# The second mixture of experts of an attention and two-MoE kernel: routing, folding of the weights, and staging

## The reference, cut to what matters

```
c = exp(logits - logits.max(1)); c /= c.sum(1)        # 3072 x 32
x = c @ slot_out                                      # soft MoE, 3072 x 512
logits = x @ w_gate                                   # 512 x 8
expert_idx = argmax(logits, axis=1)
gate_w = softmax(logits)[arange(N), expert_idx]
for e in range(8):
    mask = expert_idx == e
    if not mask.any(): continue
    out[mask] = gate_w[mask, None] * (np.maximum(x[mask] @ w1[e], 0) @ w2[e])
```

## Time and profile before

| | |
|---|---|
| median of 3 runs | 523.89 us (521.55 to 524.42) |
| the profiled execution | 521.48 us |
| its span, first to last instruction | 519.4 us |
| TensorE busy | 472.0 us (91%) |
| VectorE, ScalarE, GpSimd busy | 236.9, 222.9, 203.8 us |
| mean granted TensorE clock | 0.951 of full |
| read from HBM, written | 94.11 MB, 8.13 MB |

### The profile page before, as it was taken

The page is one execution under the profiler, slowest core; times in us unless marked ns, Lnnn a source line. Parts: engine busy times, 40 slices in busy tenths (PEclk is TensorE's granted clock), DMA queues, the critical chain, the costliest instruction groups (busy, mean ns, idle before and its releaser), DMA issues. The chain is left out here.

```text
span 519.4 us, 9980 instructions
## 1 busy us (share of the span) xinstructions
PE 472.0 (91%) x3247; PEld 378.9 (73%) x3248; DVE 236.9 (46%) x783; ACT 222.9 (43%) x442; POOL 203.8 (39%) x183
## 2 busy tenths in 40 slices
PE   8799999999999799899958997579999999999962
PEld 8599999999999777455524242458888888888842
DVE  5467777777777534631112950413333333333352
ACT  1578778778777443210101766412222222222231
POOL 2888888898985001010000001013333333333312
PEclk9999999999999989989995999679999999999977
DMA  6599899867651096599999960443333333333321
GB/s 235 207 414 387 317 370 333 334 236 261 232 190 59 8 368 278 212 392 401 408 415 409 410 229 5 130 169 128 130 132 131 131 132 131 131 132 131 130 66 49
DMA packets 38069, 116.37 MB, mean 224 GB/s; under 512 B 4304, under 2 KB 4304, under 8 KB 38032
## 3 DMA queue, kind: packets, MB, share of 16 engines
q1 hardware_dynamic: 27104, 92.28, 46.9%
q10 hardware_dynamic: 7632, 13.90, 6.9%
q0 software_dynamic: 3296, 9.70, 5.4%
HBM read 94.11 MB, written 8.13 MB: 197 GB/s over the span
## 5 line engine op out<-in xcount | busy, mean ns | idle before, releaser
L431 ACT ACTIVATE Pb<-Pb,nm 128x256 f32<-128x256 f32 (+1 forms) x192 | 83.7, 484 | 33.3 <-DVE nm L532 33.3
L378 PE MATMUL O<-V,PTs 128*128 128x65 f32 x704 | 90.2, 269 | 1.1 <-ACT PTs L457 1.1
L1335 PE MATMUL Gp<-w2h,hh 128*128 128x512 f32 x200 | 85.8, 429 | 5.8 <-DVE w2l L1570 4.9
L378 PEld LDWEIGHTS O<-V,PTs 128*128 128x128 f32 x704 | 86.4, 191 | 2.4 <-ACT PTs L457 1.3
L532 DVE CUSTOM_DVE_ANT_0 Pb<-S,TA 128x256 f32<-128x256 f32 (+1 forms) x192 | 68.7, 396 | 36.4 <-PE S L351 34.4
L1336 PE MATMUL Gp<-w2l,hh 128*128 128x512 f32 x200 | 80.3, 401 | 0.0
L1337 PE MATMUL Gp<-w2h,hl 128*128 128x512 f32 x200 | 80.2, 401 | 0.0
L1386 ACT ACTIVATE hh<-Gp 128x512 fp32r<-128x512 f32 x51 | 30.6, 600 | 109.2 <-PE Gp L1290 104.3
L1214 POOL DMA_INDIRECT Cg<-c_rows,src x28 | 27.5, 984 | 102.3 <-PE Cp L1284 100.5
L309 POOL TENSOR_TENSOR kl<-k_raw,kh 128x1632 fp32r<-128x1632 f32 x15 | 55.2, 3681 | 8.5 <-ACT kh L441 8.3
L360 PE MATMUL PT<-ident,Pb 128*128 128x128 f32 x352 | 55.2, 275 | 2.1 <-ACT Pb L431 2.1
(11 more groups left out here) (229 smaller groups left out, 655.2 us busy)
## 6 DMA issues: line engine op xcount, KB each, us to landing
mem<-in_moe_w SPq DMA_DIRECT2D x20, 2048.0 KB, 14.1
Gst<-Gall ACTq DMA_DIRECT2D x53, 256.0 KB
k_raw<-in_k SPq DMA_DIRECT2D x16, 816.0 KB, 8.2
q_raw<-in_q SPq DMA_DIRECT2D x16, 768.0 KB, 6.7
ext<-in_moe_w SPq DMA_DIRECT2D x6, 2048.0 KB, 17.9
V<-in_v SPq DMA_DIRECT2D x16, 715.0 KB, 5.4
c_rows<-XL POOLq DMA_DIRECT2D x1, 1536.0 KB, 13.8
Cg<-c_rows,src POOLq DMA_INDIRECT x28
```

Of the source, the lines that this page charges most:

```text
L378: mm = pe.matmul(O[grp % 2][:, at:at + VC], PTs[:, par, (h * kbs + kb) * P:(h * kbs + kb + 1) * P], V[:, buf, h, vb, :], start=(n == 0), s ...
L431: nc.scalar.activation(Pb[:, par, h, 0:width(g)], Pb[:, par, h, 0:width(g)], ACT.Exp, bias=nm[:, par, h:h + 1], scale=-1.0).then_inc(exp_d ...
L1335: pe.matmul(Y, hh[:, fc, :], w2h[:, cols], start=(fc == 0), stop=False)
```

## The change

Folding is moved behind the routing and done only for the experts that have tokens, from the list of them. SP loads no v1 in the soft block; when the list is known it loads the v1 of each active expert into one of two slots, then the first w2. Folding uses full matmuls that add the four chunks up in PSUM, with the replicated `STR`, so joining and its copy fall away, and the low rows are made by VectorE from PSUM. G is kept by the rank of the expert, and comes to the stage by ScalarE copies instead of DMAs. Counts come from column sums before the matmul (8 columns instead of 192), running sums from scans. The sort is two passes, first the token index, later the two gate columns; `OB` is made in 24 operations, and `OB` and `OW` have buffers of their own. The first three gathers take their index without a copy. `busy(n)` are n matmuls of 128 columns whose result nobody reads. A tiny load of w_gate only serves the semaphore count.

```diff
-        for e in range(XSLOTS - 1 + MEMW):
-            sp.wait_ge(piece_used, MEMW + EXT + e + 1)
-            load_v1(sp, e)
...
+        busy(3)
         pe.wait_ge(y_out, 1)
...
         mm.then_inc(st_done, 1)
+        busy(3)
...
-    Gall = sb(st, "Gall", [P, NE, F], F32R)
+    Gall = mem[:, 2:4, :].rearrange("p a (b f) -> p (a b) f", f=F)
-    OB = w2l[:, 0:TT * P].rearrange("p (t c) -> p t c", c=P)
-    OW = w2h[:, 0:TT * 3 * MAXT].rearrange("p (t a b) -> p t a b", a=3, b=MAXT)
+    OB = sb(st, "OB", [P, TT, P], F32R)
+    OW = sb(st, "OW", [P, TT, 3, MAXT], F32R)
...
+    def v1_slot(r):
+        return mem[:, MEMW + r, :] if isinstance(r, int) else mem[:, bass.ds(MEMW + r, 1), :].rearrange(
+            "p a f -> p (a f)")
+    def load_v1(sp, e, r, done):
+        sp.dma_start(v1_slot(r).rearrange("p (c f) -> p c f", c=DC),
+                     v1_d[bass.ds(e, 1)].rearrange("a (c p) f -> p (a c) f", p=P)).then_inc(done, 16)
     @block.sync
     def _(sp):
-        for e in range(2):
-            sp.wait_ge(gp_done, 2 * e + 2)
-            load_v1(sp, NE - 2 + e)
-        sp.wait_ge(gp_done, 6)
-        sp.wait_ge(rt_ready, 1)
-        load_v2(sp, entry(sp, 0, 0))
+        sp.dma_start(spare[:, 0:DC * NE].rearrange("p (c s) -> p c s", c=DC),
+                     wg_d.rearrange("(c p) s -> p c s", p=P)).then_inc(v1_rest, 16)
+        sp.wait_ge(experts_known, 1)
+        load_v1(sp, entry(sp, 0, 0), 0, v1_first)
         used = count(sp)
         with sp.If(used > 1):
             with sp.Fori(1, used) as r:
                 e = entry(sp, r, 0)
+                sp.wait_ge(v1_rest, r * 16)
+                sp.sem_inc(sp_passed, 1)
+                sp.wait_ge(gp_done, r * 2)
+                sp.sem_inc(sp_passed, 1)
+                load_v1(sp, e, r % 2, v1_rest)
+        load_v2(sp, entry(sp, 0, 0))
+        with sp.If(used > 1):
+            with sp.Fori(1, used) as r:
+                e = entry(sp, r, 0)
                 sp.wait_ge(w2_low, r * W2CH)
                 sp.sem_inc(sp_passed, 1)
                 load_v2(sp, e)
...
+        pool.sem_inc(gp_done, 2)
+        pool.sem_inc(g_low, 2)
         pool.wait_ge(src_ready, 1)
         def gather(u, turned):
...
-            nc.gpsimd.tensor_copy(src1[:], src_i[:, bass.ds(column(u), 1)]).then_inc(src_copied, 1)
-            pool.wait_ge(src_copied, u + 1)
+            if isinstance(u, int):
+                index = src_i[:, u:u + 1]
+            else:
+                index = src1[:, 0:1]
+                nc.gpsimd.tensor_copy(src1[:], src_i[:, bass.ds(column(u), 1)]).then_inc(src_copied, 1)
+                pool.wait_ge(src_copied, u - 2)
...
             nc.gpsimd.indirect_dma_start(out=Cg[:], out_offset=None, in_=c_dram,
-                                         in_offset=bass.IndirectOffsetOnAxis(ap=src1[:, 0:1], axis=0)
+                                         in_offset=bass.IndirectOffsetOnAxis(ap=index, axis=0)
                                          ).then_inc(gathered, 16)
         for u in range(3):
             gather(u, u)
+        pool.wait_ge(rt_ready, 1)
+        pool.wait_ge(dst_ready, 1)
...
+        def busy(count):
+            for _ in range(count):
+                pe.matmul(Cp[:, 0:P], ident[:], ones[:], start=True, stop=True)
+        def sort(which, cols):
+            for t in range(TT):
+                if t % REP == 0:
+                    pe.wait_ge(hot_done, t // REP + 1)
+                mm = pe.matmul(Sp[:, cols], OB[:, t, :], OW[:, t, which].rearrange("p a b -> p (a b)"),
+                               start=(t == 0), stop=(t == TT - 1))
+            mm.then_inc(sorted_done, 1)
...
         mm.then_inc(gw_done, 1)
+        busy(3)
         pe.wait_ge(gw_out, 1)
...
         mm.then_inc(l2_done, 1)
-        pe.wait_ge(nident_done, 1)
-        units(range(0, 2))
+        busy(9)
         pe.wait_ge(oh_done, 1)
         pe.wait_ge(lt_done, 1)
-        pe.matmul(Rp, lt[:], oh[:].rearrange("p t e -> p (t e)"), start=True, stop=True)
-        pe.matmul(Tp, ones[:], oh[:].rearrange("p t e -> p (t e)"),
-                  start=True, stop=True).then_inc(ranks_done, 1)
-        units(range(2, 2 * (NE - 2)))
-        for t in range(TT):
-            if t % REP == 0:
-                pe.wait_ge(hot_done, t // REP + 1)
-            mm = pe.matmul(Sp[:, 0:3 * MAXT], OB[:, t, :], OW[:, t].rearrange("p a b -> p (a b)"),
-                           start=(t == 0), stop=(t == TT - 1))
-        mm.then_inc(sorted_done, 1)
-        units(range(2 * (NE - 2), UNITS + 2))
+        pe.matmul(Rp, lt[:], cnt[:], start=True, stop=True)
+        pe.matmul(Tp, ones[:], cnt[:], start=True, stop=True).then_inc(ranks_done, 1)
+        busy(28)
+        sort(slice(0, 1), slice(0, MAXT))
+        pe.wait_ge(v1_first, 16)
+        used = count(pe)
+        with pe.Fori(0, used) as r:
+            pe.wait_ge(v1_rest, (r + 1) * 16)
+            pe.wait_ge(g_low, r * 2 + 2)
+            slot = v1_slot(r % 2)
+            for half in range(2):
+                for c in range(DC):
+                    at = c * F + half * 512
+                    mm = pe.matmul(Gp[:, half, :], STR[:, c].rearrange("p r s -> p (r s)"), slot[:, at:at + 512],
+                                   start=(c == 0), stop=(c == DC - 1))
+                mm.then_inc(gp_done, 1)
         turn(0)
         pe.wait_ge(cgt_out, 1)
+        pe.wait_ge(g_low, used * 2 + 2)
         for half in range(2):
             hidden(0, half)
-        with pe.Fori(0, count(pe)) as rank:
+        pe.wait_ge(gates_hot, 1)
+        sort(slice(1, 3), slice(MAXT, 3 * MAXT))
+        pe.wait_ge(rt_ready, 1)
+        with pe.Fori(0, used) as rank:
...
+        act.wait_ge(r_shifted, 1)
+        nc.scalar.activation(E2[:], T2[:], ACT.Exp).then_inc(r_exp, 1)
+        act.wait_ge(experts_known, 1)
+        used = count(act)
+        with act.Fori(0, used) as r:
+            for half in range(2):
+                act.wait_ge(gp_done, r * 2 + half + 3)
+                nc.scalar.copy(Gall[:, bass.ds(r, 1), half * 512:(half + 1) * 512].rearrange(
+                    "p a f -> p (a f)").bitcast(F32R), Gp[:, half, :]).then_inc(g_high, 1)
...
         def fetch(e, half):
             cols = slice(half * 512, (half + 1) * 512)
-            act.dma_start(Gst[:, cols].bitcast(F32),
-                          Gall[:, bass.ds(e, 1), cols].rearrange("p a f -> p (a f)").bitcast(F32)).then_inc(g_here[half], 16)
+            g = Gall[:, e, cols] if isinstance(e, int) else Gall[:, bass.ds(e, 1), cols].rearrange("p a f -> p (a f)")
+            nc.scalar.copy(Gst[:, cols], g).then_inc(g_here[half], 1)
         act.wait_ge(rt_ready, 1)
-        act.wait_ge(g_low, 2 * NE)
-        e0 = act.value_load(te[0:1, 0:1], min_val=0, max_val=NE - 1)
-        for half in range(2):
-            fetch(e0, half)
-        act.wait_ge(v2_loaded, 16)
-        act.wait_ge(sorted_done, 1)
-        for ch in range(W2CH):
+        e1 = act.value_load(tr[0:1, 1:2], min_val=0, max_val=NE - 1)
+        act.wait_ge(g_low, used * 2 + 2)
+        act.sem_inc(act_passed, 1)
+        def second_high(ch):
+            act.wait_ge(v2_loaded, 16)
             nc.scalar.copy(w2h[:, chunk(ch)], raw[:, chunk(ch)]).then_inc(w2_high, 1)
+        fetch(0, 0)
         turned_out(0)
-        e1 = act.value_load(te[0:1, 1:2], min_val=0, max_val=NE - 1)
+        fetch(0, 1)
+        second_high(0)
         relu(0, 0)
         fetch(e1, 0)
-        used = count(act)
+        for ch in range(1, W2CH):
+            second_high(ch)
...
-        total = all_tiles(act)
-        for half in range(2):
-            act.wait_ge(g_here[half], (total + 2 - half) * 16)
-        act.sem_inc(act_passed, 1)
...
+        dve.wait_ge(gw_done, 1)
+        v.tensor_tensor(GWs[:], GWp.unsqueeze(1).to_broadcast([P, REP, NE]),
+                        own_rows[:].unsqueeze(2).to_broadcast([P, REP, NE]), ALU.mult).then_inc(gw_out, 1)
...
         dve.wait_ge(l2_done, 1)
+        L2 = L2p.rearrange("p (t e) -> p t e", e=NE)
+        step(v.tensor_reduce(m2[:], L2, AX, ALU.max))
+        v.tensor_tensor(T2[:], L2, over_experts(m2[:]), ALU.subtract).then_inc(r_shifted, 1)
         dve.wait_ge(r_shifted, 1)
+        step(v.scalar_tensor_tensor(T1[:], T2[:], 0.0, over_tiles(ex[:]), ALU.is_equal, ALU.mult))
         step(v.tensor_reduce(m2[:], T1[:], AX, ALU.min))
+        step(v.tensor_tensor(by_tile(oh[:]), over_experts(m2[:]), over_tiles(ex[:]), ALU.is_equal))
+        v.tensor_reduce(cnt[:], oh[:], AX, ALU.add).then_inc(oh_done, 1)
+        v.tensor_tensor_scan(flat(cum[:]), flat(keep[:]), flat(oh[:]), 0.0, ALU.mult, ALU.add)
         dve.wait_ge(ranks_done, 1)
+        v.tensor_scalar(nt_i[:, 0, :], Tp, float(P - 1), None, ALU.add)
+        step(v.tensor_scalar(act[:], Tp, 0.0, None, ALU.is_gt))
+        v.tensor_scalar(nt_i[:, 1, :], nt_i[:, 0, :], 7, None, ALU.logical_shift_right)
+        step(v.tensor_tensor_scan(order[:], keep[:, 0, 1:1 + NE], act[:], 0.0, ALU.mult, ALU.add))
...
```

(38 more changed lines are left out.)

222 lines of the change are left out of this document (53 added, 169 removed).

## The result

The median is 505.08 us (four runs, 501.17 to 507.07) against 524.15 us (four runs, 521.55 to 528.09) before, a ratio of 0.962 with an interval of 0.953 to 0.971. Run again in five rounds, the changed kernel has 502.97 us against 523.92, a ratio of 0.959 (0.953 to 0.965); one of these six runs, 506.50, counts as slow and is left out of the ratio. So the change makes the kernel faster, by 19 to 21 us between medians; 26 us in the span and 27 between medians had been forecast.

What follows compares the result with a forecast made beforehand. Bounds named: the soft-MoE barrier, folding all eight experts and the loop's entry, then TensorE's 6.49 us tile pitch. Loop start 309.3 + 1.7 first tile + 2.7 clock = 313.7, against 339.9, saves 26.2: span 493.2, forecast 496.5 us, range 491 to 505.

Steps and rivals of the forecast that it cites:

- Block end: End of the soft MoE: without the six v1 loads the barrier follows VectorE at 268.8 us, saving 5.5.
- router: From the block's end to the list of experts: steps sum to 7.8 us, experts known at 276.6, not 293.4.
- Load: First expert's v1 after the list: 7.6 us from issue to landing, landed at 285.05.
- Sorting beside it: VectorE's positions, one-hot products and OB during the load: OB 3.6 us, index pass ends at 285.1, level with the load.
- rival (b): Chain of list, load and fold longer than priced, by slow landing or OB pieces of 0.21: 500 to 503 us; chance 0.15.
- This change escapes: Cutting OB into 24 pieces avoids the skill's fixed-cost warning: 0.13 us a piece by its table, 3.0 in all.
- Fold: Two listed experts on TensorE: 6.9 us each with 1.5 after each, both G's whole at 302.75.
- Entry of the loop: From folded weights to the tile loop: ScalarE 4.6 us, VectorE 1.2 and 0.7; loop starts at 309.3.
- First tile: First tile of the loop: w2 chunks and register loads delay it, ending near 317.5 instead of 315.8; loss 1.7 us.
- Clock: Granted clock falling ahead of the fold and ahead of the loop: an allowance of 2.7 us.
- Rival (a): Clock lost for most of the fold: 509 to 511 us at half clock throughout, 503 with half of it; chance 0.10.
- Stage copies: ScalarE's two copies of 0.58 us replacing two DMA issues of 0.5 in the steady loop, costed at nothing.

Runs made afterwards that it cites:

- Experiment 1: Kernel before the change, with only the fifth and sixth v1 loads moved from the soft block to the head of the last block: 518.39 us against 525.69.
- experiment 7: Changed kernel with the old packed fold (four products on 32 columns, one joining matmul), only for the listed experts: 495.35 us, ratio 0.946 to before.
- experiment 9: Changed kernel with OB made by six operations of 512 columns instead of 24 of 128: 499.68 us.
- Experiment 6: Changed kernel with TensorE's second sorting pass (gates) moved ahead of the wait for the first stage of G: 503.84 us against 502.97.
- experiment 3: Changed kernel with the stage of G filled by DMAs from ScalarE's queue again instead of copies: 505.71 us.
- experiment 10: Changed kernel with two idle matmuls ahead of each of the six groups of the index sorting pass: 502.47 us.

## Why the prediction was right, and where its size was off

The direction, the order of the steps and the bound after the change were right: SP was early at the barrier, the loop waits for no DMA into the stage, the pitch is still 6.49 us (17 tiles between 362.23 and 472.57). The forecast of 496.5 was 8.6 us below the first median and 6.5 below the second; the first, 505.08, lies 0.1 us above the upper end of the range, the second inside. The terms of the sum, by the time since the stretch's start:

- **Block end** (5.5 forecast) and **router**: right. The list was known 10.42 us after the stretch's start; 276.6 - 266.57 = 10.03 had been forecast. Experiment 1 gives the block end by itself, with the clock that it keeps, 7.3.
- **Load**: SP's first load landed 7.9 us after its issue (7.6 forecast). But it was not the bound.
- **Sorting beside it** was the step that failed first. The fold started 21.36 us into the stretch, not 19.4: 2.0 us. The list was 0.4 late, the positions took 2.9 us for 2.5, and OB 4.78 for 3.6, which is 1.2 of the 2.0. OB had been put at 0.15 a piece, "near the 0.17 of a small one": the pieces start every 0.20 us and last 0.277. "Three operations of 0.39" was also too low for two of them, which take 0.62 and 0.63 through the exchanged axes; a row of the kernel before could have shown it, L1523 with 0.59. The 1.25 us from the end of OB to the fold are about what had been forecast (284.8 to 285.95), and experiment 7, with the same pass and OB but the clock whole up to 291.5, has 1.23 (291.30 to 292.53), so the half clock in the index pass cost next to nothing. The late start is rival (b), by its second half and not by a slow landing. The cycle table of the Trainium skill (VectorE: DVE Perf Modes, section on the TRN2 errata) had been given as 0.13 us a piece by estimate; the trace has 0.20, so its warning of a fixed cost per small operation was the part to weigh. The same section says that the 58 cycles are too few for the length of a single operation, where about 150 were measured, and the estimate had left that out. "This change escapes" was wrong: the 24 pieces took 1.09 us more than the six wide operations of experiment 9 (4.78 against 3.69). If both ways paid one price, 3.69 / 6 for 512 columns and 4.78 / 24 for 128 would make it, by estimate, 1.08 ns a column and 0.06 us an operation.
- **Fold**: 6.9 an expert was 7.13, 1.5 between was 1.87, each small; the first expert at partly half clock 8.55. With the start, the folded weights are whole 4.4 us later than forecast.
- **Entry of the loop**: 6.5 forecast, 7.96 measured, from VectorE's last subtraction (its end at 310.60) to 318.56. "TensorE's second sorting pass is under this" held at full clock alone; at half it took 5.27 and ended last. Experiment 6 gives back 1.37 of it by moving the pass: the forecast chain of ScalarE and VectorE stands only that far behind.
- **First tile**: 1.7 forecast, and from 318.56 on the loop lost 1.8. The number is right by luck. The register loads that were to hold the relu of the second half did not: it follows the w2 chunks without a wait. 1.45 of the loss is the half clock, 4.36 us (318.56 to 322.92) for the 2.91 of the earlier trace rows.
- **Clock**: 2.7 had been allowed, half of a fall ahead of the fold and most of one ahead of the loop. Both falls came: 1.4 in the first expert (8.55 - 7.13), up to 1.4 at the loop's entry, and the 1.45 of the first half tile, together 4.3. Rival (a), the clock lost for most of the fold, did not come.
- **Stage copies** at nothing in the steady loop: right. Their value at the entry was overrated: experiment 3 gives them 2.1 us, where the stall of 8.74 (3.5 on TensorE) had been counted as theirs.

In numbers: the new loop, taken back without losses from 472.57, would have begun 472.57 - 2.91 - 23 x 6.49 - 270.03 = 50.4 us into the stretch; forecast was 313.7 - 266.57 = 47.1. The 3.2 between them are 4.4 (weights whole later) + 1.4 (entry) + 0.1 (first tiles) - 2.7 (the clock's allowance, which these terms contain), and they are the difference of 26.2 and 22.95.

The rest, from 23 down to 20 between the two profiles, lies ahead of the stretch. The code there is the same but for the six loads that are gone and three idle matmuls. The baseline was a favourable one: its profiled execution, 521.48 us at a mean granted clock of 0.951, is like only 3 of the 29 runs of before in the later sessions (518.96 to 521.41 us at 0.950 to 0.953); the other 26 took 520.21 to 526.89 us at 0.932 to 0.941. What makes the clock fall in the attention in some executions was not looked into, and so why the medians, too, differ by less than the stretch stays open.

## What to carry to other kernels

When work is cut from a loop, price the new unit beside the old one: here a unit became twice as dear (8.98 for 4.56 us), the cut from eight to two hid it, and giving the cheap form back was worth another 7.5 us. Look at the engine that issues DMAs when a barrier comes: moving two loads behind it gained 7 us with no work removed. And ask what follows the place where idle matmuls keep the clock: here a wait of about two microseconds stood behind it (1.87 us between the experts), and experiment 10 only moved the fall from one expert to the next.

## What the runs showed of the hardware that had not been expected

- A VectorE operation with two tensors of 192 elements takes 0.36 us with matching axes, 0.62 to 0.63 when one operand or the result goes through exchanged axes (24 elements apart), and 0.59 in the kernel before (L1523). A plain copy out of PSUM through exchanged axes (L1475 of before) took 0.36, so this does not hold for every operation.
- A compare of 128 x 128 against a scalar per partition is 0.277 us long and starts every 0.20 us; six operations on 512 columns did the same work in 3.69 instead of 4.78 us (experiment 9).
- A scan over 192 elements takes 0.55 us, 1.5 times a tensor_tensor of that size. The Trainium skill (DVE: opcode table, instruction layouts, handler registers and perf-mode slots, section Datapath and trigger behaviour) says half throughput, and the estimate of 0.56 from it was met.
- The granted clock of the changed kernel fell at 287.5 us, after TensorE had waited 1.3 us for OB and then run matmuls of 34 columns with short waits between. But in experiment 7 the same instructions after the same wait (1.28 us) ran at whole clock from 287.4 to 291.5, and the fall came then. Counted from the stretch's start, the place of the fall moved by 2.8 us between two executions of the same code, and one profile does not show what brought it.
- DMAs of a stage half between places of SBUF land in 2.3 us in the median of experiment 3, and one took 8.74 us beside a w2 load.
